# Attention on one core: keys read in place instead of through copied windows, fp32 logits in column groups, output rows gathered in SBUF and stored in 2 KB rows

## The chip, the core and the metric

The kernel runs on one core of a Trainium2 chip. The metric is the device time of one execution, in microseconds; lower is better. Engines are named as in the profile: PE (TensorE matmul), PEld (its weight loads), DVE (VectorE), ACT (ScalarE), POOL (GpSimd), SP (SyncE, which issues most DMAs here).

## What is computed

Three stages in one launch. Inputs are fp32, batch 4, 8 heads, 768 positions, head dimension 64, 8 memory keys and values a head.

```python
for c in range(768 // 32):                       # chunks of 32 queries
    k_full = concat(mem_k, k[c*32-16 : c*32+40]) # clipped at both ends
    scores = scale * q_c @ k_full.T; a = softmax(scores); out[c] = a @ v_full
x = out.transpose(0, 2, 1, 3).reshape(3072, 512)
do = x @ w_skip > 0                              # first expert stage, only these rows
e = argmax(x @ w_gate); y = gate * relu(x @ w1[e]) @ w2[e]; x = x + y
h = max(x @ v1, x @ v2, x @ v3); result = h @ w_out   # final stage, 768 wide
```

## The kernel before

**Attention.** Two heads stand on the 128 partitions, so a batch has 4 pairs (PAIRS). A pair has 768 queries: 6 tiles of 128, taken 3 at a time (TPG); such a group is one step of the pipeline, 8 steps a batch (GPB), 32 in all. Step s does, each on its engine and behind semaphores: scores of group s (PE L1034), edge mask, row maximum and subtraction (DVE L761, L764, L766), exp (ACT L629); for group s-1 the turning of the probabilities (PE L1049), their copy to probT (ACT L612), the values product (PE L1082), and on DVE the normalising (L795, L797, L801) into `xn`; for group s-2 the turning of xn (PE L1067), its split into a high part (ACT L617) and a low part (DVE L787), and the store of xn to x_dram (ACT's queue, L623); for group s-3 the logits product (PE L1060, L1061) with an 18-column weight of high and low parts. The PE order within a step is scores(s), turn prob(s-1), logits(s-3), turn xn(s-2), values(s-1). Once a batch, logits are copied (DVE L783), turned in six pieces (L1015) and summed over their two halves (DVE L749).

A score matmul has 32 queries as weights and writes 32 PSUM partitions; its moving operand is the window of both heads, 2 x 64 keys (16 left, 32 own, 8 right, 8 memory). The windows overlap, so keys are loaded to `k_raw` and copied into `k_sb`: head 0 by DVE (first half of the chunks) and POOL (second half), head 1 by ACT, in three copies each (lay_left, lay_right, L356 to L361). The other head's half of k_sb and v_sb is zero, written once: k_sb by DVE (L737 to L741), v_sb by ACT (`clear`).

**Queues.** SP loads keys one pair ahead (L382, behind the copies of the pair two back), queries (L385) and values (two DMAs, L401, behind the values product of the pair two back), with two buffers of each. The store of xn is issued by ACT in 512-byte rows, 192 KB a group, 32 in all; L800 makes DVE wait, before it writes xn, for the store of the group two back. Behind attention SP loads final weight blocks 0 and 1 (L409, EARLY), the expert chunks (L423) once the routing table stands, and the gate values.

**Routing and experts.** DVE turns the logits into a table and slot numbers (L830 to L893), POOL gathers rows of x_dram (L532), a loop over 256-row tiles follows (L1135 to L1137, split fp32 as three fp32r products), and POOL scatters the rows back (L583). ACT and DVE split weights (L654, L665, L916, L928).

**Final stage.** SP loads rows (L443, L444) and the weight blocks 2 to 5; six groups of 512 rows follow.

```python
if not isinstance(b, int) or n >= 2:          # L799, DVE
    dve.wait_ge(s_xst[g % 2], b * (16 * GPB // 2) + 16 * ((s - 1) // 2))
act.dma_start(dst[:, :, j * P:(j + 1) * P], xn[g % 2]...)   # L623
```

Of the kernel before, what the change touches and what calls it, by code (L numbers as in the profile page):

```python
# [6 lines left out]
F32 = mybir.dt.float32  # L7
F32R = mybir.dt.float32r
# [6 lines left out]
P = 128  # L15
# [3 lines left out]
WIN = LEFT + CHUNK + RIGHT + MEM  # L19
# [7 lines left out]
LOGS = LAG + 1  # L27
PADK = LEFT + S + RIGHT + MEM
GCH = NCH // GROUPS
# [14 lines left out]
W18 = 2 * (E + 1)  # L44
# [16 lines left out]
EARLY = 2  # L61


def pipeline(eng, step, ahead=False):

    for s in range(GPB):
        step(0, s)
    with eng.Fori(1, B - 1 if ahead else B) as b:  # L70
        for s in range(GPB):
            step(b, s)
    for s in range(0 if ahead else GPB, GPB + LAG):
        step(B - 1, s)


def behind(b, s, k):

    if s - k >= GPB or (isinstance(b, int) and b * GPB + s - k < 0):
        return None  # L80
    return (s - k) % GPB, b * GPB + (s - k)


def build(nc, qT, kT, vW, w9, wpack, wfin, out):
# [6 lines left out]
    with ctx:  # L91
# [12 lines left out]
        with ExitStack() as landing:  # L104

            sb, _ = tensors(landing)
            fin_raw = sb("fin_raw", [P, FB2, FC])
        sb, _ = tensors(ctx)
# [20 lines left out]
        with ExitStack() as att:  # L129
            sb, ps = tensors(att)  # L130
            q_sb = [sb(f"q_sb{i}", [P, S]) for i in range(2)]
            k_raw = [sb(f"k_raw{i}", [P, PADK]) for i in range(2)]
            k_sb = [sb(f"k_sb{i}", [P, 2, NCH, WIN]) for i in range(2)]
            v_sb = [sb(f"v_sb{i}", [P, 2, NCH, DV]) for i in range(2)]
            prob = [sb(f"prob{i}", [P, TPG, 2, WIN]) for i in range(2)]
            probT = sb("probT", [P, TPG, P])
            xn = [sb(f"xn{i}", [P, TPG, 2, D]) for i in range(2)]
            xT_hi = sb("xT_hi", [P, GW], F32R)
            xT_lo = sb("xT_lo", [P, GW], F32R)
# [3 lines left out]
            w9_sb = sb("w9_sb", [P, KD, E + 1])  # L143
            w18 = sb("w18", [P, KD, W18], F32R)
            zero = sb("zero", [P, 1])
            part = sb("part", [W18, S])
            ps_s = [ps(f"ps_s{i}", [P, TPG, 2, WIN]) for i in range(2)]

            ps_pT = ps("ps_pT", [P, GW + S // P * W18])
            ps_o = [ps(f"ps_o{i}", [P, TPG, 2, DV]) for i in range(2)]  # L150
            ps_xT = ps("ps_xT", [P, GW])
            ps_part = [ps(f"ps_part{i}", [P, GW]) for i in range(GROUPS)]
# [81 lines left out]
        s_zt = sem("s_zt")  # L234
        s_zk = sem("s_zk")
        s_zv0 = sem("s_zv0")
        s_zv1 = sem("s_zv1")
        s_w9 = sem("s_w9")
        s_q = [sem(f"s_q{i}") for i in range(2)]
        s_k = [sem(f"s_k{i}") for i in range(2)]  # L240
        s_kw = sem("s_kw")
        s_kwv = sem("s_kwv")
        s_kwa = sem("s_kwa")
        s_v = [sem(f"s_v{i}") for i in range(2)]
# [4 lines left out]
        s_carry = sem("s_carry")  # L249
# [12 lines left out]
        s_xst = [sem(f"s_xst{i}") for i in range(2)]  # L262
        s_xT = sem("s_xT")
        s_xThi = sem("s_xThi")
        s_xTlo = sem("s_xTlo")
# [4 lines left out]
        s_whi18 = sem("s_whi18")  # L270
        s_w18 = sem("s_w18")
# [58 lines left out]
        x_g = x_dram.rearrange("(b u t p) c -> b u p t c", b=B, u=GROUPS, p=P)  # L330
# [23 lines left out]
        def lay_left(copy, n, rows, head, lo, hi):  # L354
            keys = k_raw[n][:, :].rearrange("p (c w) -> p c w", w=CHUNK)
            return copy(k_sb[n][rows, head, lo:hi, 0:CHUNK], keys[rows, lo:hi, :])  # L356

        def lay_right(copy, n, rows, head, lo, hi):
            keys = k_raw[n][:, :].rearrange("p (c w) -> p c w", w=CHUNK)
            copy(k_sb[n][rows, head, lo:hi, CHUNK:WIN - MEM], keys[rows, lo + 1:hi + 1, 0:WIN - MEM - CHUNK])  # L360
            return copy(k_sb[n][rows, head, lo:hi, WIN - MEM:],  # L361
                        k_raw[n][rows, PADK - MEM:].unsqueeze(1).to_broadcast([D, hi - lo, MEM]))
# [5 lines left out]
        def _(sp):  # L368
            def one(x, b):

                return x[b] if isinstance(b, int) else x[bass.ds(b, 1)].rearrange("a p c -> (a p) c")

            def older(b, j):

                return not isinstance(b, int) or b * PAIRS + j >= 2

            def load_k(b, j):
                if older(b, j):
                    sp.wait_ge(s_kw, b * PAIRS + j - 1)
                    sp.wait_ge(s_kwa, b * PAIRS + j - 1)  # L380
                    sp.wait_ge(s_kwv, b * PAIRS + j - 1)
                sp.dma_start(k_raw[j % 2][:, :], one(kT[:, j % PAIRS], b + j // PAIRS)).then_inc(s_k[j % 2], 16)  # L382

            def load_q(b, j):
                sp.dma_start(q_sb[j % 2][:, :], one(qT[:, j], b)).then_inc(s_q[j % 2], 16)  # L385

            def load(b, s):
                j, n = s // GROUPS, s // GROUPS % 2
                if s >= GPB or s % GROUPS:
                    return  # L390

                if not (isinstance(b, int) and b == B - 1 and j == PAIRS - 1):
                    load_k(b, j + 1)
                if older(b, j):
                    sp.wait_ge(s_score, b * GPB + s - 2 * GROUPS + GROUPS)
                if not (isinstance(b, int) and b == 0 and j == 0):
                    load_q(b, j)
                if older(b, j):
                    sp.wait_ge(s_o, b * GPB + s - 2 * GROUPS + GROUPS)
                for h in range(2):  # L400
                    sp.dma_start(v_sb[n][D * h:D * h + D, h, :, :], one(vW[:, j, h], b)).then_inc(s_v[n], 16)  # L401

            load_k(0, 0)
            load_q(0, 0)
            sp.dma_start(w9_sb[:, :, :], w9).then_inc(s_w9, 16)
            pipeline(sp, load, ahead=True)
# [4 lines left out]
            sp.wait_ge(s_xn, B * GPB)  # L411
            for n in range(2):
                sp.wait_ge(s_xst[n], 16 * B * GPB // 2)
            for f in range(EARLY):
                load_fin(f)
# [61 lines left out]
        def _(pool):  # L477
# [12 lines left out]
            def windows(b, s):  # L490
                if isinstance(b, int) and b * GPB + s == 1:
                    routing_constants()
                if s >= GPB or s % GROUPS:
                    return
                j, n = s // GROUPS, s // GROUPS % 2
                pool.wait_ge(s_k[n], b * (16 * PAIRS // 2) + 16 * (j // 2 + 1))
                if not isinstance(b, int) or b * PAIRS + j >= 2:
                    pool.wait_ge(s_score, b * GPB + s - 2 * GROUPS + GROUPS)
                order()
                lay_left(pool.tensor_copy, n, slice(0, D), 0, GCH, NCH)  # L500
                lay_right(pool.tensor_copy, n, slice(0, D), 0, GCH, NCH).then_inc(s_kw, 1)
# [13 lines left out]
            pipeline(pool, windows)  # L515
            pool.wait_ge(s_logc, B)
            for n in range(2):
                pool.wait_ge(s_xst[n], 16 * B * GPB // 2)
# [8 lines left out]
            pool.wait_ge(s_route, 1)  # L527
            pool.wait_ge(s_clr, 2)
# [63 lines left out]
        def _(act):  # L592
# [3 lines left out]
            def clear(x, rows, head):  # L596
                return act_copy(x[rows, head].rearrange("p c d -> p (c d)"), zero[rows, :].to_broadcast([D, NCH * DV]))

            def windows(b, s):

                j, n = s // GROUPS, s // GROUPS % 2
                act.wait_ge(s_k[n], b * (16 * PAIRS // 2) + 16 * (j // 2 + 1))
                if not isinstance(b, int) or b * PAIRS + j >= 2:
                    act.wait_ge(s_score, b * GPB + s - GROUPS)
                lay_left(act_copy, n, slice(D, P), 1, 0, NCH)
                lay_right(act_copy, n, slice(D, P), 1, 0, NCH).then_inc(s_kwa, 1)

            def attend(b, s):
                if at := behind(b, s, 1):
                    g, n = at  # L610
                    act.wait_ge(s_pT, n + 1)
                    act.activation(probT[:, :, :].rearrange("p t c -> p (t c)"), ps_pT[:, 0:GW], ACT.Copy)\  # L612
                        .then_inc(s_pTc, 1)
# [656 lines left out]
```

## Time and profile before

| what | value |
|---|---|
| median of 3 runs | 780.99 us (779.65 to 781.51) |
| the profiled execution | 783.93 us, its span 782.2 us |
| PE busy | 725.0 us, 93% of the span |
| DVE, ACT, POOL busy | 352.6, 260.2, 115.6 us |
| mean granted clock of TensorE | 0.969 of full |
| moved | 91.35 MB; packets under 2 KB: 17644 of 40525 |

Line numbers are those of the kernel before. A fp32 matmul of the attention's scores and values products is two records in the trace (768 for 384 matmuls). Attention fills 0 to about 136 us of the span, routing up to about 160, the expert loop up to about 356, the final stage the rest. A row of a timeline gives start, duration, engine, line, what is written from what, shapes, the number of merged instructions, and in brackets the idle time before and what ended it.

### The profile page before, as it was taken

The page shows a single profiled execution, that of the slowest core. Times are in us where ns is not written, and L with a number is a line of the kernel's source. Part 1 is how long each engine was busy: PE and PEld are TensorE (multiplying, and loading weights), DVE is VectorE, ACT ScalarE, POOL GpSimd, SP SyncE. Part 2 cuts the span into 40 slices and gives each one's busy share as a digit, 9 for nine tenths or more (in the row PEclk, how much of TensorE's full clock was granted, in tenths as well). Part 3 has the DMA queues.
Part 4 walks back from the last instruction along what each step waited for, and adds up shares of the span by engine and source line. Part 5 has one row for each costly group of instructions (what it writes and reads, how often), then busy time and mean ns, then how long its engine had stood idle before and what let it go on. Part 6 is the DMA issues. An engine that isn't in the chain of part 4 may idle for free.

```text
span 782.2 us, 13009 instructions
## 1 busy us (share of the span) xinstructions
PE 725.0 (93%) x4946; PEld 596.5 (76%) x4947; DVE 352.6 (45%) x648; ACT 260.2 (33%) x414; POOL 115.6 (15%) x161
## 2 busy tenths in 40 slices
PE   4877877489999999997999999999999999999998
PEld 3665655389999999985888888888888888888886
DVE  6776887856665666662432222222222122222212
ACT  6665664245555555542321111111111111111101
POOL 3111110141545434641000000000000000000000
PEclk9999999589999999997999999999999999999999
DMA  8899895566667656637100200020030002001001
GB/s 227 222 275 264 249 287 138 193 204 198 202 211 230 205 193 208 182 110 286 44 1 1 107 1 1 11 97 1 0 108 0 0 0 107 0 0 54 1 0 54
DMA packets 40525, 91.35 MB, mean 117 GB/s; under 512 B 5356, under 2 KB 17644, under 8 KB 39728
## 3 DMA queue, kind: packets, MB, share of 16 engines
q1 hardware_dynamic: 24400, 79.67, 33.1%
q10 hardware_dynamic: 12800, 6.29, 2.8%
q0 software_dynamic: 3296, 5.00, 1.9%
q8 instruction: 19, 0.31, 0.2%
q14 instruction: 10, 0.08, 0.0%
HBM read 78.08 MB, written 16.79 MB: 121 GB/s over the span
## 4 chain that ended last, share of the span: by engine, by line
PE 81%; DMA 9%; DVE 6%; ACT 2%; issue 2%; POOL 0%; SPq 0%; ACTq 0%; DVEq 0%; POOLq 0%
PE ps_m L1135 13%; PE ps_m L1137 13%; PE ps_m L1136 13%; DMA x_dram<-xn 6%; PE ps_f L1137 4%; PE ps_f L1136 4%; PE ps_f L1135 4%; PE ps_h L1135 4%; PE ps_h L1136 4%; PE ps_h L1137 4%; PE ps_y L1135 4%; PE ps_y L1136 4%; PE ps_y L1137 4%; PE ps_fx L1179 1%; DMA q_sb<-qT 1%
## 5 line engine op out<-in xcount | busy, mean ns | idle before, releaser
L1135 PE MATMUL ps_m<-f_xhi,fin_lo 128*128 128x512 f32 x432 | 171.5, 397 | 1.4 <-DVE f_xlo L966 1.4
L1137 PE MATMUL ps_m<-f_xhi,fin_hi 128*128 128x512 f32 x432 | 171.3, 397 | 0.0
L1136 PE MATMUL ps_m<-f_xlo,fin_hi 128*128 128x512 f32 x432 | 171.3, 396 | 0.0
L916 DVE TENSOR_TENSOR w_lo<-raw,w_hi 128x1024 fp32r<-128x1024 f32 x67 | 82.9, 1238 | 62.4 <-ACT w_hi L665 62.4
L976 DVE TENSOR_TENSOR f_b<-ps_m,f_a 128x512 f32<-128x512 f32 x36 | 24.9, 692 | 181.7 <-PE ps_m L1137 181.6
L1135 PEld LDWEIGHTS ps_m<-f_xhi,fin_lo 128*128 128x128 f32 x432 | 81.6, 189 | 21.4 <-DVE f_xlo L966 1.8
L1136 PEld LDWEIGHTS ps_m<-f_xlo,fin_hi 128*128 128x128 f32 x432 | 81.6, 189 | 19.7
L1137 PEld LDWEIGHTS ps_m<-f_xhi,fin_hi 128*128 128x128 f32 x432 | 81.5, 189 | 19.8
L701 ACT ACTIVATE f_hhi<-f_h 128x512 fp32r<-128x512 f32 x36 | 22.8, 632 | 206.7 <-DVE f_h L979 206.7
L665 ACT ACTIVATE w_hi<-raw 128x1024 fp32r<-128x1024 f32 x67 | 70.9, 1058 | 56.4 <-PE ps_y L1137 50.5
L1135 PE MATMUL ps_h<-x_hi,w_lo 128*128 128x256 f32 x256 | 73.4, 287 | 2.2 <-DVE x_lo L923 2.2
L1136 PE MATMUL ps_h<-x_lo,w_hi 128*128 128x256 f32 x256 | 73.5, 287 | 0.0
L1137 PE MATMUL ps_h<-x_hi,w_hi 128*128 128x256 f32 x256 | 73.4, 287 | 0.0
L699 ACT ACTIVATE f_a<-ps_m 128x512 f32<-128x512 f32 x36 | 21.5, 596 | 113.9 <-PE ps_m L1137 113.9
L979 DVE TENSOR_TENSOR f_h<-ps_m,f_b 128x512 f32<-128x512 f32 x36 | 24.9, 692 | 75.9 <-PE ps_m L1137 75.9
L1135 PE MATMUL ps_f<-fin_hi,f_hlo 128*128 128x512 f32 x144 | 58.4, 405 | 0.0
L1137 PE MATMUL ps_f<-fin_hi,f_hhi 128*128 128x512 f32 x144 | 56.8, 394 | 0.0
L1136 PE MATMUL ps_f<-fin_lo,f_hhi 128*128 128x512 f32 x144 | 56.7, 394 | 0.0
L1135 PEld LDWEIGHTS ps_h<-x_hi,w_lo 128*128 128x128 f32 x256 | 50.0, 195 | 4.8 <-issue 2.4
L1136 PEld LDWEIGHTS ps_h<-x_lo,w_hi 128*128 128x128 f32 x256 | 50.0, 195 | 2.2
L1135 PE MATMUL ps_y<-w_hi,h_lo 128*128 128x512 f32 x128 | 51.3, 400 | 0.0
L1136 PE MATMUL ps_y<-w_lo,h_hi 128*128 128x512 f32 x128 | 50.5, 394 | 0.0
(158 smaller groups left out, 1033.6 us busy)
## 6 DMA issues: line engine op xcount, KB each, us to landing
raw<-wpack SPq DMA_DIRECT2D x67, 512.0 KB, 4.2
v_sb<-vW SPq DMA_DIRECT2D x32, 390.0 KB, 5.8
k_raw<-kT SPq DMA_DIRECT2D x16, 400.0 KB, 6.3
q_sb<-qT SPq DMA_DIRECT2D x16, 384.0 KB, 6.5
x_dram<-xn ACTq DMA_DIRECT2D x32, 192.0 KB, 4.1
fin_raw<-wfin SPq DMA_DIRECT2D x6, 1024.0 KB, 11.0
f_in<-x_dram SPq DMA_DIRECT2D x5, 1024.0 KB, 5.5
out<-f_out SPq DMA_DIRECT2D x5, 1024.0 KB, 4.2
```

The source lines that it names most:

```text
L665: act.activation(w_hi[c % RING][:, :], raw[:, c % RAW, :], ACT.Copy).then_inc(s_whi, 1)
L699: act.activation(f_a[:, :], ps_m[0][:, :], ACT.Copy).then_inc(s_fa, 1)
L701: act.activation(f_hhi[f % 2][:, :], f_h[:, :], ACT.Copy).then_inc(s_fhhi, 1)
L916: dve.tensor_tensor(w_lo[c % RING][:, :], raw[:, c % RAW, :], w_hi[c % RING][:, :].bitcast(F32), ALU.subtract).then_inc(s_wlo, 1)
L976: dve.tensor_tensor(f_b[:, :], ps_m[1][:, :], f_a[:, :], ALU.max).then_inc(s_fb, 1)
L979: dve.tensor_tensor(f_h[:, :], ps_m[2][:, :], f_b[:, :], ALU.max).then_inc(s_fh, 1)
L1135: pe.matmul(out_, a_lo, b_hi, start=first, stop=False)
L1136: pe.matmul(out_, a_hi, b_lo, start=False, stop=False)
L1137: return pe.matmul(out_, a_hi, b_hi, start=False, stop=end)
L1179: last = pe.transpose(ps_fx[:, t * P:(t + 1) * P], f_in[par][:, t, k * P:(k + 1) * P], ident[:, :])
```

## The change

- Keys: no k_raw and no copies. k_sb holds the 800 raw columns of both heads (the other head's rows zero). A score is two matmuls, one over 2 x 56 keys read in place, one over 2 x 8 memory keys. Keys land by two DMAs of 64 partitions.
- Three buffers of q, k, v (SETS) instead of two. SP issues all loads in order, keys and queries of the next pair behind the values of this one.
- Output: DVE writes the normalised rows into `x_buf`, which holds all of x (24 tiles of 512 columns). SP stores it once a batch, 1.5 MB, batches 0 to 2 after all loads of attention, then final weight block 0, then batch 3. No store on ACT's queue, and no wait of DVE for one.
- Logits: xT is copied once by ACT in fp32, with no low part. Three matmuls (one a tile) with a 32-column weight, each to its own 32 PSUM partitions. They are copied, turned in one piece and copied to `logits` once a group of the last pair, 8 times.
- POOL clears v_sb and then writes the routing constants; ACT does no clearing. The loops over batches are unrolled.
- Waits on the stores move: POOL before the gather, ACT before its first final split (x_buf and fin_hi share their place). Final block 1 is loaded behind the first rows of the final stage.

```diff
-            q_sb = [sb(f"q_sb{i}", [P, S]) for i in range(2)]
-            k_raw = [sb(f"k_raw{i}", [P, PADK]) for i in range(2)]
-            k_sb = [sb(f"k_sb{i}", [P, 2, NCH, WIN]) for i in range(2)]
+            q_sb = [sb(f"q_sb{i}", [P, S]) for i in range(SETS)]
+            k_sb = [sb(f"k_sb{i}", [P, 2, PADK]) for i in range(SETS)]
...
+            def load_qk(n):
+                b, j, i = n // PAIRS, n % PAIRS, n % SETS
+                if n >= SETS:
+                    sp.wait_ge(s_score, (n - SETS + 1) * GROUPS)
+                for h in range(2):
+                    sp.dma_start(k_sb[i][D * h:D * h + D, h, :], kT[b, j, D * h:D * h + D, :]).then_inc(s_qk[i], 16)
+                sp.dma_start(q_sb[i][:, :], qT[b, j]).then_inc(s_qk[i], 16)
+
+            def load_v(n):
+                b, j, i = n // PAIRS, n % PAIRS, n % SETS
+                if n >= SETS:
+                    sp.wait_ge(s_o, (n - SETS + 1) * GROUPS)
+                for h in range(2):
+                    sp.dma_start(v_sb[i][D * h:D * h + D, h, :, :], vW[b, j, h]).then_inc(s_v[i], 16)
+
+            def store_x(b):
+                sp.wait_ge(s_xn, (b + 1) * GPB)
+                sp.dma_start(x_b[b], x_buf[:, b * (S // P):(b + 1) * (S // P), :]).then_inc(s_xst, 16)
...
+            load_qk(0)
+            sp.dma_start(w9_sb[:, :, :], w9).then_inc(s_w9, 16)
+            for n in range(NPAIR):
+                load_v(n)
+                if n + 1 < NPAIR:
+                    load_qk(n + 1)
+            for b in range(B - 1):
+                store_x(b)
+            load_fin(0)
+            store_x(B - 1)
...
+            load_fin(1)
             sp.dma_start(f_in[1][:, :, :], x_f[1]).then_inc(s_fin[1], 16)
-            for f in range(EARLY, FB2):
+            for f in range(2, FB2):
...
+            pool.wait_ge(s_xst, 16 * B)
             pool.wait_ge(s_clr, 2)
...
-                    act.activation(xT_hi[:, :], ps_xT[:, :], ACT.Copy).then_inc(s_xThi, 1)
+                    act_copy(xT[:, :], ps_xT[:, :]).then_inc(s_xTc, 1)
...
+            act.wait_ge(s_xst, 16 * B)
             split_fin(0)
...
-                    dve.wait_ge(s_xThi, n + 1)
-                    dve.tensor_tensor(xT_lo[:, :], ps_xT[:, :], xT_hi[:, :].bitcast(F32), ALU.subtract)\
-                        .then_inc(s_xTlo, 1)
...
-                    if not isinstance(b, int) or n >= 2:
-                        dve.wait_ge(s_xst[g % 2], b * (16 * GPB // 2) + 16 * ((s - 1) // 2))
...
-                            last = pe.matmul(ps_s[g % 2][CHUNK * r:CHUNK * (r + 1), t, :, :],
-                                             q_sb[j % 2][:, c * CHUNK:(c + 1) * CHUNK],
-                                             k_sb[j % 2][:, :, c, :], start=True, stop=True)
+                            queries = q_sb[i][:, c * CHUNK:(c + 1) * CHUNK]
+                            rows = slice(CHUNK * r, CHUNK * (r + 1))
+                            pe.matmul(ps_s[n % 2][rows, t, :, 0:KEYS], queries,
+                                      k_sb[i][:, :, c * CHUNK:c * CHUNK + KEYS], start=True, stop=True)
+                            last = pe.matmul(ps_s[n % 2][rows, t, :, KEYS:], queries,
+                                             k_sb[i][:, :, PADK - MEM:], start=True, stop=True)
...
-                    pe.matmul(ps_part[u][0:W18, :], w18[:, j, :], xT_lo[:, :], start=(j == 0), stop=False)
-                    pe.matmul(ps_part[u][0:W18, :], w18[:, j, :], xT_hi[:, :], start=False,
-                              stop=(j == PAIRS - 1)).then_inc(s_part, 1)
+                    for t in range(TPG):
+                        last = pe.matmul(ps_part[u][t * W9:(t + 1) * W9, 0:P], w9_sb[:, j, :], xT[:, t * P:(t + 1) * P],
+                                         start=(j == 0), stop=(j == PAIRS - 1))
+                    last.then_inc(s_part, 1)
```

## Rows read from the trace of the kernel before

**Rows 1.** The page's part 4: chain that ended last, by engine
```profile
PE 81%; DMA 9%; DVE 6%; ACT 2%; issue 2%; POOL 0%; SPq 0%; ACTq 0%; DVEq 0%; POOLq 0%
```

**Rows 2.** The chain in 20 to 136 us: by line; start, us, what
```profile
by line: DMA x_dram<-xn 41.4%; issue 7.1%; ACT k_sb L594 7.1%; DVE xn L801 5.1%; PE ps_xT L1067 4.5%; DVE smax L764 4.4%; PE ps_s L1034 4.4%; DVE prob L766 3.9%; PE ps_o L1082 3.7%; DVE xT_lo L787 3.4%; PE ps_pT L1049 3.0%; ACT xT_hi L617 1
...
70.09 7.91 DMA x_dram<-xn
```

**Rows 3.** Groups by line, DVE, 0 to 136 us: busy, mean ns, idle
```profile
L801 DVE TENSOR_TENSOR xn<-ps_o,srec 128x384 f32<-128x384 f32 x32 | 17.8, 558 | 15.7 <-DMA x_dram<-xn 14.4
...
L787 DVE TENSOR_TENSOR xT_lo<-ps_xT,xT_hi 128x384 fp32r<-128x384 f32 x32 | 17.5, 546 | 3.4 <-ACT xT_hi L617 3.2
```

**Rows 4.** Queues in 0:20, 20:60, 60:120, 120:134: packets, MB, engine share
```profile
q1 hardware_dynamic: 1468, 4.43, 83.6%
...
q1 hardware_dynamic: 2242, 8.02, 73.8%
q10 hardware_dynamic: 4175, 2.06, 18.0%
...
q1 hardware_dynamic: 3442, 12.40, 75.9%
q10 hardware_dynamic: 6625, 3.25, 18.5%
...
q1 hardware_dynamic: 160, 0.80, 25.8%
```

**Rows 5.** Busy by window: five engines, PE clock, DMA share, GB/s
```profile
50.00:60.00 10.00, 8.58 (x174) 6.50 (x174) 8.63 (x28) 6.86 (x13) 1.20 (x4) 1.00 1.01 282
```

**Rows 6.** Timeline of PE, 33 and 116 to 127 us: start, us, what
```profile
33.01 1.52 PE L1034 MATMUL ps_s<-k_sb,q_sb 128*32 128x128 f32 x24
...
116.50 0.55 PE L1015 MATMUL ps_pT<-ident,part 18*128 18x18 f32 x6
...
122.20 0.86 PE L1034 MATMUL ps_s<-k_sb,q_sb 128*32 128x128 f32 x24
...
124.84 0.84 PE L1034 MATMUL ps_s<-k_sb,q_sb 128*32 128x128 f32 x24
125.61 0.55 PE L1049 MATMUL ps_pT<-ident,prob 128*128 128x128 f32 x3
125.91 0.42 PE L1060 MATMUL ps_part<-xT_lo,w 128*18 128x384 f32 x1
...
126.83 0.87 PE L1082 MATMUL ps_o<-v_sb,probT 128*32 128x130 f32 x24
```

**Rows 7.** Groups by line, PE, 115 to 127 us: busy, mean ns
```profile
L1034 PE MATMUL ps_s<-k_sb,q_sb 128*32 128x128 f32 x96 | 3.4, 272 | 0.0
...
L1015 PE MATMUL ps_pT<-ident,part 18*128 18x18 f32 x6 | 0.5, 214 | 0.0
```

**Rows 8.** Timeline of the start: weights of the first values product
```profile
13.13 1.09 PEld L1082 LDWEIGHTS ps_o<-v_sb,probT 128*32 128x32 f32 x24 [1.70 <-DMA v_sb<-vW]
```

**Rows 9.** Timeline from the logits to the first expert product
```profile
135.38 0.27 DVE L749 TENSOR_REDUCE logits<-ps_pT 128x54 f32<-128x108 f32 x1 [0.98 <-PE ps_pT L1015]
...
135.71 0.95 POOL L520 MEMSET x_in<- 128x1024 f32 x1 [22.44 <-DVE logits L749]
...
151.72 1.21 POOL L532 DMA_INDIRECT x_in<-x_dram,idx_g  x1 [0.29 <-POOL idx_g L537]
...
159.84 0.57 PE L1135 MATMUL ps_h<-x_hi,w_lo 128*128 128x256 f32 x1 [2.19 <-DVE x_lo L923]
```

**Rows 10.** The page's part 6, DMA issues: count, KB each, us to landing
```profile
fin_raw<-wfin SPq DMA_DIRECT2D x6, 1024.0 KB, 11.0
...
out<-f_out SPq DMA_DIRECT2D x5, 1024.0 KB, 4.2
```

**Rows 11.** Timeline of ACT at the start of the final stage
```profile
364.68 1.90 ACT L654 ACTIVATE fin_hi<-fin_raw 128x2048 fp32r<-128x2048 f32 x1
370.57 0.60 ACT L699 ACTIVATE f_a<-ps_m 128x512 f32<-128x512 f32 x1 [3.99 <-PE ps_m L1137]
```

More of the change, by code:

```diff
@@ L26 @@
 LAG = 3
-LOGS = LAG + 1
+STEPS = B * GPB
+NPAIR = B * PAIRS
+SETS = 3
 PADK = LEFT + S + RIGHT + MEM
-GCH = NCH // GROUPS
 GW = TPG * P
@@ L60, with pipeline @@
 NIX = 2
[L61 to L81, printed above, removed]
+def pipeline(step):
+    for s in range(STEPS + LAG):
+        step(s)
 def build(nc, qT, kT, vW, w9, wpack, wfin, out):
@@ L261, in build @@
         s_xn = sem("s_xn")
-        s_xst = [sem(f"s_xst{i}") for i in range(2)]
+        s_xst = sem("s_xst")
         s_xT = sem("s_xT")
-        s_xThi = sem("s_xThi")
-        s_xTlo = sem("s_xTlo")
+        s_xTc = sem("s_xTc")
         s_part = sem("s_part")
@@ L352, in first_rows, with where, spot @@
             return x[:, :, t * P:(t + 1) * P]
[L354 to L362, printed above, removed]
+        def where(n):
+            return n // GPB, n % GPB // GROUPS, n % GROUPS
+        def spot(n):
+            return n // GPB * (S // P) + n % GROUPS * TPG
         block = ctx.enter_context(nc.Block())
@@ L513, in routing_constants @@
                               allow_small_or_imprecise_dtypes=True).then_inc(s_rc, 1)
[L515 to L518, printed above, removed]
+            pool.wait_ge(s_const, 1)
+            for i in range(SETS):
+                for h in range(2):
+                    if 2 * i + h > 0:
+                        pool.wait_ge(s_zv, 2 * i + h)
+                    pool.memset(v_sb[i][D * h:D * h + D, 1 - h, :, :], 0.0).then_inc(s_zv, 1)
+            pool.wait_ge(s_zv, 2 * SETS)
+            routing_constants()
+            pool.wait_ge(s_logc, B * GROUPS)
             pool.memset(x_in[:, :, :], 0.0).then_inc(s_clr, 1)
@@ L644, in _ @@
-            act.wait_ge(s_w9, 16)
-            act.activation(w18[:, :, 0:E + 1], w9_sb[:, :, :], ACT.Copy).then_inc(s_whi18, 1)
-            clear(v_sb[1], slice(0, D), 1)
-            pipeline(act, attend, ahead=True)
+            pipeline(attend)
             act.wait_ge(s_ldiff, 1)
@@ L752, in attend @@
-            def attend(b, s):
-                if at := behind(b, s, 0):
-                    g, n = at
+            for i in range(SETS):
+                for h in range(2):
+                    dve.memset(k_sb[i][D * h:D * h + D, 1 - h, :], 0.0).then_inc(s_zk, 1)
+            def copy_logits(n):
+                dve.wait_ge(s_log, n + 1)
+                dve.tensor_copy(logits[:, n * TPG:(n + 1) * TPG, :],
+                                ps_part[n % GROUPS][:, P:].rearrange("p (t e) -> p t e", e=W9)[:, :, 0:E + 1])\
+                    .then_inc(s_logc, 1)
@@ L789, in attend @@
-                if s == LOGS and not (isinstance(b, int) and b == 0):
-                    copy_logits(b)
-                if at := behind(b, s, 1):
-                    g, n = at
+                if 0 <= (n := s - 3) < STEPS:
+                    b, j, u = where(n)
+                    if j == PAIRS - 1:
+                        dve.wait_ge(s_part, n + 1)
+                        dve.tensor_copy(part[:, u, :], ps_part[u][0:TPG * W9, 0:P]).then_inc(s_partc, 1)
+                if 0 <= (n := s - 1) < STEPS:
+                    b, j, u = where(n)
```

299 lines of the change are left out of this document (89 added, 210 removed).

## The prediction

> **What bounds the kernel now.** I read the chain of work that ended last first. Over the whole span it is 81% matmul and 9% DMA [rows 1]; the matmuls belong to the two expert stages after about 160 us, and the change leaves their code alone. So the gain or loss must come from the attention stage, 0 to 136 us, and from what it hands on. The same chain, cut to 20 to 136 us, is another picture: 41.4% of it is the store of normalised rows, `x_dram<-xn`, in pieces of up to 7.91 us [rows 2]. With two `xn` buffers, the multiply of group n (L801) waits until the store of group n-2 has landed: DVE stands 14.4 us before it [rows 3].
>
> Why does a 192 KB store take 6 to 8 us? The queues answer. In 20 to 60 us the loads (q1) take 73.8% of the 16 engines and the stores (q10) 18.0%; in 60 to 120 us 75.9% and 18.5% [rows 4]. In 50 to 60 us their busy share is 1.01, at 282 GB/s [rows 5]. **The DMA engines are nearly full, and a small store queues among big loads.** The chain names the store's latency; the resource behind it is engine time. That decides the estimate: removing the wait can bring the stage down to the engine time of its loads, and no further.
>
> **What the loads need.** Their engine time is 83.6% of 20 us, 73.8% of 40, 75.9% of 60 and 25.8% of 14 [rows 4]: 16.7 + 29.5 + 45.5 + 3.6 = 95.3 us. Bytes of q, k and v are the same afterwards. The stores take 18.0% of 40 and 18.5% of 60, 18.3 us up to 120, and some 3 more behind; three quarters of them now go behind the last load, the rest behind those. Loads start at about 2 us and can hold the engines full, since the first three pairs (SETS = 3) wait for nothing and later ones only for a pair three back. So the last values land at about 2 + 95.3 = 97 us, and the last keys and queries, ahead of that half pair of bytes, at about 94 to 95.
>
> **What the compute needs.** In the one stretch without store waits, score bursts start at 122.20 and 124.84: 2.64 us a group [rows 6]. Inside it two hand-offs lock the step: from 125.61 to 126.83 PE turns prob, ACT copies it to probT, and the values product may start (1.22); the values burst follows, and the next score burst. The parts:
> - Scores: 12 matmuls over 128 columns become 24, over 112 and 16. Each fp32 matmul is two records: 24 records become 48. The four 32-column groups run side by side now: a record of 128 columns takes 0.27 us, and 24 take 0.84 [rows 6, 7]. Total columns stay, so the low end of the cost is zero. The nearest row for a small fp32 matmul is the turn of `part` (L1015, 18 columns, six in 0.55 us, one 0.21): (0.55 - 0.21) / 5, about 68 ns each [rows 6, 7]. Over four column groups at once, six added records each, that is 0.41 us, less the 0.07 that the shorter key matmuls give back: 0.34. L1015 loads 128 weight columns, these 32, so I take 0.25. The high end is all 24 added records one after another, 1.63 us.
> - Logits: one pair of 384-column matmuls (L1060 and L1061; the record of the first alone is 0.42 us [rows 6]) becomes three matmuls in three column groups, six records of 128 columns; two rounds of about 0.11 us, 0.25 with the hand-over. PE gains 0.2 us, but that stretch lies beside ACT's probT copy, which sets the start of the values product: nothing on the path.
> - DVE loses xT_lo, 0.546 us a group [rows 3], and its key copies; it gets logits copies 8 times instead of 4, small ones. ACT loses its key copies and the 32 store issues. Neither engine then has 2.6 us of work in a group. POOL's copies go too. All of that is hidden under PE and DMA and counts zero; it only makes the 2.64 safe.
> - SP loses all waits for copied windows (three semaphores) and gains the four stores of x, placed behind all loads. What queues behind a store's wait on SP is the first final weight block, then the first expert chunks, due later.
> So a group costs 2.64 + 0.25 = 2.89 us of compute, against 95.3 / 32 = 2.98 us of DMA. **DMA is the bound by a little**, and compute follows the loads.
>
> **The start.** The first values product came at 13.13, waiting for v, which stood behind the next pair's keys in the queue [rows 8]. Now the scores wait for k, q and two memsets, no window copies (about 5 us, an estimate), and v(0) comes directly behind: about 9.5. POOL clears v_sb instead of ACT: by x_in's 0.95 us for 1024 columns [rows 9], 1.45 us each, two before the first product, all six by 11 us: hidden by the loads. Pair 1 lands at about 12.
>
> **The sum.** Last pair's scores at 95, the last group's at 98. From the last score burst (124.84) to the end of the logits reduction (135.38 + 0.27) is 10.8 us now [rows 6, 9]; without xT_lo, with a copy of 128 instead of 384 columns and one turn of logits instead of six, about 9.5. That gives 107.5; I add 2 us for loads that don't pack perfectly: logits at **109.5** instead of 135.65, 26.1 us earlier. Routing (135.65 to the gather at 151.72, 16.1 us) and the way on to the first expert product (159.84) are the same code [rows 9]. Everything behind shifts, if the stores don't hold it.
>
> **The stores of x.** SP reaches them near 87 us; they flow from 97. Three of 1.5 MB, 1 MB of final weights, and the last 1.5 MB: some 7.3 MB. At 282 GB/s [rows 5] they need 26 us and end at 123. The gather is due at 109.5 + 16.1 = 125.6: 2.6 us of slack. At the 4.2 us to landing that a 1 MB store has [rows 10], one by one, it would be 128, 2 us late; that is an upper bound, since these overlap. I count zero and keep 2 to 5 us for the range. ACT now waits for these stores before it splits the first final block; then come 1.9 us and three splits of half the elements each, about 1 us, to about 128, before the first expert product (109.5 + 24.2 = 133.7).
>
> **The final stage.** Final block 1 now lands behind f_in[0], and such a block takes 11.0 us from issue to landing among others [rows 10], that is about 368.5 on the old clock. Its split (1.90 us, at 364.68 now) stands in front of f_a at 370.57, which has 4.0 us of idle before it [rows 11]: it just fits. Zero, and 1 us for the range.
>
> The profiled execution took 783.93 us; 783.93 - 26.1 = 757.8. It lies 2.9 above the median of the runs, so I predict 780.99 - 26.1 = **754.9, rounded 755**. Its own range, with 0 to 0.34 us a group for the small matmuls and loads 6% better or worse, is 750 to 761.
>
> **Rivals.**
> (1) *The score burst is paced by its records, not its columns.* 24 records in 0.84 us, less the 0.27 of one, are 25 ns each [rows 6, 7]; that fits a fixed pace too. Then 48 records add 0.6 us, a group costs 3.24, and from pair 1 at 12 us the last score burst is at 12 + 29 x 3.24 = 106, logits at 115 to 117: gain 19 to 21, 761. For it: those rows alone don't separate the two readings. Against it: a burst at the lower clock took 1.52 us [rows 6], nearly twice as long, as column work must and a fixed pace of issue needn't. Chance 0.2.
> The Trainium skill has this rule (TensorEngine Tiling (Array Packing), Instruction Overhead): every matmul carries about 60 cycles, so one column costs as much as sixty, and splitting a dimension that is already small doesn't pay. By it the 24 small records cost an estimated 25 ns each, 0.6 us a group if they line up, and the result is this rival's 761; spread over four column groups it would be 0.15, within my term.
> (2) *Slower: the small matmuls serialise.* If each record of the memory matmuls holds up its column group's neighbours for L1015's 68 ns, the score burst grows by 1.6 us, a group takes 4.27, the last score burst comes at 12 + 29 x 4.27 = 136 and the logits at 145: about 10 us later than now, 791. The turn is at 3.94 us a group, 54 ns for each added record. For it: L1015 is the only small fp32 matmul in the trace. Against it: it loads four times the weight columns, in no column group. Chance 0.06.
> (3) *The DMA bound stays or moves.* Keys now land by two DMAs of 64 partitions, as v does; if the loads run 8% slower, or the stores come 5 us late for the gather, the gain is 18 to 21: 760 to 763. Chance 0.12.
> (4) *Nothing comes of it*: the stage is bound by something that I don't see, and stays within 2 us. Chance 0.03.
> The forecast has the remaining 0.59.
>
> **How the numbers follow.** The range 749 to 768 holds the forecast, rivals 1 and 3 with some room, and leaves out 2 and 4. Faster by over 0.3% (2.3 us, about what this kernel's measurement can tell from no change): 0.91; within it 0.03; slower 0.06.
>
> **What would show it.** DMA share near 1.0 from 3 to 97 us with no stores in it; no L801 wait on a DMA; PE waiting for q, k or v at pair starts; a score burst of 0.9 to 1.2 us (1.4 means rival 1, over 2 rival 2); groups at 2.9 to 3.0 us; logits ready at 107 to 112; the gather with no wait for stores; the expert stages as long as before. PE without idle through the stage, at over 3.1 us a group, would say that compute and not DMA is the bound, and my term for the small matmuls is wrong. A span of expert stages that differs by over 2 us would be a cause that I haven't counted.

## The result and the profile after

The change made the kernel slower: 797.9 us (median of 4 runs, 793.3 to 800.3) against 781.3 for the kernel before on the same chip, a ratio of 1.019 [1.012, 1.027]. 755 was predicted, and the range ended at 768. The page of the changed kernel's profiled execution (793.31 us, the shortest of the four, 4.6 below their median), its span, PE's busy time and the DMA queues:

```profile
span 791.5 us, 14338 instructions
...
PE 731.7 (92%) x5827; PEld 605.0 (76%) x5827; DVE 325.1 (41%) x572; ACT 224.8 (28%) x361; POOL 109.3 (14%) x119
...
q1 hardware_dynamic: 27792, 86.01, 36.2%
...
q8 instruction: 33, 0.54, 0.3%
...
q_sb<-qT SPq DMA_DIRECT2D x16, 384.0 KB, 7.6
```

q8 is of the kind "instruction". The page of the kernel before has for it:

```profile
q8 instruction: 19, 0.31, 0.2%
```

The change writes PE's 32 attention groups out one after another where the kernel before loops over batches, and PE's compiled program grew from 313 KB to 546 KB. q8's packets are of 16 KB, and in both kernels their sum is the size of PE's program: they are its blocks, fetched.

The timeline between attention and the experts (lmax, DVE's first step on the finished logits; the gather; the first expert product) answers to [rows 9]:

```profile
146.24 0.35 DVE L716 TENSOR_REDUCE lmax<-logits 128x24 f32<-128x192 f32 x1
...
162.27 1.21 POOL L483 DMA_INDIRECT x_in<-x_dram,idx_g  x1 [0.29 <-POOL idx_g L488]
...
170.43 0.58 PE L1013 MATMUL ps_h<-x_hi,w_lo 128*128 128x256 f32 x1 [2.20 <-DVE x_lo L807]
```

The same DVE step (L830 there) began at 135.69 before. So the logits are done 10.6 us **later**, not 26 earlier. From there on nothing differs much: 16.0 us to the gather and 8.2 to the first product, as before, and the 9.3 us by which the span is longer are these 10.6 less 1.3 behind. In this execution the whole loss is in attention; where the other 4.6 us of the median lie, no trace shows.

Now PE's timeline there. One group is as forecast; the next is cut in two:

```profile
65.09 0.41 PE L909 MATMUL ps_s<-k_sb,q_sb 128*32 128x112 f32 x8
...
66.02 0.55 PE L921 MATMUL ps_pT<-ident,prob 128*128 128x128 f32 x3
...
67.32 0.87 PE L956 MATMUL ps_o<-v_sb,probT 128*32 128x130 f32 x24
68.02 0.40 PE L909 MATMUL ps_s<-k_sb,q_sb 128*32 128x112 f32 x6
68.20 0.24 PE L911 MATMUL ps_s<-k_sb,q_sb 128*32 128x16 f32 x4
70.01 0.18 PE L911 MATMUL ps_s<-k_sb,q_sb 128*32 128x16 f32 x1 [1.56 <-issue]
```

The reader is to see two things. From burst to burst it is 68.02 - 65.09 = 2.93 us, against my 2.89; the burst to the turn of prob takes 0.93, against 0.77 before (124.84 to 125.61 [rows 6]): 24 added records cost 0.16 us. Then PE stops in the middle of a burst for 1.56 us, with its operands in place. "issue" is idle time for which the profile shows no releaser. PE's rows of this kind in the waits of 0 to 150 us:

```profile
PE ps_s L909 <- issue: 9.1, 5, 2.9
PE ps_s L911 <- issue: 6.0, 3, 3.1
PE ps_o L956 <- issue: 5.0, 1, 5.0
PE ps_part L932 <- issue: 4.1, 3, 1.4
PE ps_pT L921 <- issue: 2.1, 1, 2.1
```

They sum to 26.3 us. In the trace's packets the 16 KB fetches of q8 come every 4 to 9 us from 27 to 141 us and take 0.9 to 1.5 us each. Of PE's 13 stops of over 1 us behind 18 us, nine begin 0.9 to 1.5 us after such a packet starts, that is about when it ends, and three more have a whole packet inside them. So the stops stand at the fetches, but what PE waits for inside one, the rest of this block or the next, the trace doesn't show. In the kernel before there were 7 fetches up to 73 us and none from there to 160. DVE's two longest waits are on PE now, none on a DMA: the store wait of [rows 3] is gone, and something took its place.

### The profile page after: what moved, and what is told of

It is laid out like the page before. It is cut to its first block, busy times and chain, and to the rows that moved or that the text cites. A ratio compares the mean times of both kernels' runs of the same rounds, so it can differ in the third digit from the quotient of the medians.

```text
span 791.5 us, 14338 instructions
## 1 busy us (share of the span) xinstructions
PE 731.7 (92%) x5827; PEld 605.0 (76%) x5827; DVE 325.1 (41%) x572; ACT 224.8 (28%) x361; POOL 109.3 (14%) x119
## 4 chain that ended last, share of the span: by engine, by line
PE 65%; DMA 2%; issue 0%; POOL 0%; DVE 0%; SPq 0%; ACT 0%; POOLq 0%; DVEq 0%
PE ps_m L1013 13%; PE ps_m L1014 13%; PE ps_m L1015 13%; PE ps_f L1015 4%; PE ps_f L1014 4%; PE ps_f L1013 4%; PE ps_y L1013 2%; PE ps_y L1014 2%; PE ps_h L1015 2%; PE ps_h L1014 2%; PE ps_y L1015 2%; PE ps_h L1013 2%; PE ps_fx L1057 1%; DMA x_in<-x_dram,idx_g 1%; DMA f_in<-x_dram 1%; PE ps_x L1007 1%
```

## The experiments

**Theory F (fetch):** written out, PE uses up 16 KB of program in fewer microseconds than a block needs to be there while q1 fills the DMA engines, and it runs dry. **Rivals:** the 24 small score records (W); the split key loads that make transfers slower (D); the three-deep load queue that makes the fetches wait (Q); and that the store part saves nothing. The kilobytes of PE's program are those of the compiled kernel; the packets of q8 bear them out (26 in e1, 22 in e5, 33 in e6). Times are medians; ratios are to the kernel before in the same batch.

### e1: the kernel before, PE's attention written out

```diff
-            pipeline(pe, attend)
+            for n in range(B):
+                for s in range(GPB):
+                    attend(n, s)
+            for s in range(GPB, GPB + LAG):
+                attend(B - 1, s)
```

> The kernel before, with PE's attention written out for all four batches instead of looping over three of them; every instruction, operand and wait is the same. PE's program grows from 313 KB to 429 KB, some 7 fetches of 16 KB more while the DMA engines are full. Theory F (PE stalls while its instructions are fetched through full DMA engines): slower by 5 to 15 us, 786 to 796, partly hidden behind the store waits. Rival W (the small matmuls and the added PE work make the change slow): no difference, 781. Rival D (the loads of the changed kernel are slower): no difference, 781.

784.0 us, 1.005 [1.001, 1.009]. A small cost, under what F had expected: either the store waits hide the gaps, or a 429 KB program is fetched in time. e11 tells these apart. PE has no row with "issue" in its attention, so even the 0.5% isn't explained by stops.

### e2: the change without its later loads

```diff
             (load_qk and load_v, from the fourth pair on)
+                    return
-                        pe.wait_ge(s_qk[i], 48 * (p // SETS + 1))
+                        pe.wait_ge(s_qk[i], 48)
```

> The changed kernel, that loads q, k and v for the first three pairs alone and uses them for all 16 (13 of 16 loads are left out); PE's program is the same to the byte. F: fetches pass an idle queue, the idle of PE put down to issue falls from about 26 us to under 8, groups take 2.9 us, 750 to 762. W: the same PE work at the same pace, 790 to 798. D predicts a gain too, but with the issue stalls still there: 785.

790.0 us, but the total can't be compared: other values route the rows differently, and 75 expert blocks are loaded instead of 67. Attention can: lmax at 117.83, 28.4 us earlier. Its queues and PE's issue rows in 20 to 110 us:

```profile
q1 hardware_dynamic: 2592, 6.19, 20.0%
q8 instruction: 19, 0.31, 1.4%
...
PE ps_s L911 <- issue: 2.6, 1, 2.6
PE ps_s L913 <- issue: 1.3, 1, 1.3
PE ps_pT L923 <- issue: 1.2, 1, 1.2
```

The same program is fetched, 19 blocks in 90 us, one in 4.7 us, and PE stops for 5.1 us; in the change it was 15 blocks and 17.5 us in the same stretch. The three stops of e2 end at 20.4 us and begin at 71.1 and 99.2: the first beside the first three pairs' loads (DMA share 1.05 in 15.0 to 20.4 us), the other two 1 and 3 us after the last packet of a stored batch of x (0.54 in 64 to 72 us, 0.53 in 96.0 to 100.5). So the fetches alone don't stall PE for long; **it takes the fetches and nearly full DMA engines together**. Part of the 28 us is also that PE no longer waits for loads, which this run doesn't separate.

### e3, e4: fewer instructions a group

e3 drops the memory keys' matmuls (12 of 128 columns a group, PE's program 447 KB). e4 computes the same as the change, but with one full-width matmul of 16 columns for each tile, 3 a group in place of 12 (472 KB):

```diff
-                            last = pe.matmul(ps_s[n % 2][rows, t, :, KEYS:], queries,
-                                             k_sb[i][:, :, PADK - MEM:], start=True, stop=True)
+                    for t in range(TPG):
+                        last = pe.matmul(ps_s[n % 2][:, t, :, KEYS:], q_sb[i][:, c:c + P],
+                                         k_sb[i][:, :, PADK - MEM:], start=True, stop=True)
```

> The changed kernel with one score matmul over 2 x 64 columns read in place (the 8 columns behind the window in place of the 8 memory keys, which are left out). 48 instructions a group less on PE, program 447 KB instead of 546 KB, 6 fetches fewer. F: 13 to 18 us faster than the change, 780 to 785, with issue stalls left. W: the whole loss and the missed gain come back, 755 to 760. D: unchanged, 797.

> The changed kernel with the memory keys of a whole tile of 128 queries in one matmul (3 of full width a group instead of 12 of 32 columns), same result. 36 instructions a group less, program 472 KB, 4.6 fetches fewer. F: 7 to 12 us faster than the change, 786 to 791. W: most of the loss back, 760 to 770. D: unchanged, 797.

e3: 773.9 us (five runs; the profiled one took 784.3, the others 768.4 to 775.4), 0.989 [0.984, 0.994], 24 us below the change where 13 to 18 were expected. 24 fewer records save some 32 x 0.16 = 5 us by their own time, an estimate; that the rest is stalls isn't shown, since the one trace is of the longest execution. It has 17.3 us of "issue" in 0 to 150 us against the change's 26.3, with a program of 7.8 KB a group, and in 20 to 110 us the DMA share of 0.99 that I had forecast for the change:

```profile
20.00:110.00 90.00, 73.43 (x1419) 50.44 (x1419) 51.36 (x153) 33.41 (x71) 0.00 (x0) 0.96 0.99 227
```

e4: 788.1 us, 1.006 [1.003, 1.010], 9.8 below the change and inside what F expected (7 to 12), though an undisturbed group takes 0.4 us longer with it. A group that is slower by itself, but has fewer bytes (8.6 KB in place of 10.9), made the kernel faster. PE's "issue" rows fell to 6.4 us, all before 73 us.

### e5, e6, e10, e7: loop or written out, the changed kernel

e5 loops PE over the batches again. With it come two load sets instead of three (a batch has four pairs), and two xn buffers into which DVE writes and which ScalarE copies into x_buf. e6 is e5 with the loop written out, and nothing else. e10 is e5 with that copy on GpSimd. e7 is the change with two sets alone.

```diff
-            pipeline(attend)
+            for s in range(GPB):
+                attend(0, s)
+            with pe.Fori(1, B) as b:
+                for s in range(GPB):
+                    attend(b, s)
```

> The changed kernel with two sets of q, k, v instead of three and PE's attention looping over batches 1 to 3, as before the change. [...] Program 371 KB instead of 546 KB. F: issue stalls after the first loop round are gone, groups of 2.9 to 3.1 us behind it, 15 to 25 us faster than e6 (the same written out). If a loop body of 86 KB doesn't stay with PE, fetches go on and there is no difference. W: no difference to e6.

> As e5, with PE's attention written out: program 546 KB, 23 fetches. F: 795 to 802. W: the same time as e5.

> The changed kernel with two sets of q, k, v instead of three, nothing else. F: the third set was worth little where PE is late, 797 to 803. Rival Q (deeper load queues make the instruction fetches wait longer): fewer issue stalls, 785 to 793. D: 800 to 806, since loads wait more.

> The change with PE's attention as a loop over batches and two sets (the run of 779.2 us), with the copy of the rows moved from ScalarE to GpSimd, which is idle in attention. Theory (that run is bound in attention by its loads and by PE's first batches, not by ScalarE): total within 2 us of 779, logits at 127 to 130. Rival (ScalarE's copy behind the last store, 7.8 us of waiting there, holds the chain up): 3 to 6 us less, 773 to 776.

e5: 779.2 us, 0.997 [0.994, 1.000]. e6: 793.3, 1.015 [1.008, 1.022]. **The same work costs 14.1 us more when PE's code is written out**, as F has it, though F had expected 15 to 25. The instruction queue and the window of 73 to 117 us, first e5, whose loop is running there, then e6:

```profile
73.00:117.00 44.00, 41.09 (x1143) 31.58 (x1146) 29.74 (x90) 24.84 (x55) 0.00 (x0) 1.00 0.99 238
```

```profile
q8 instruction: 7, 0.11, 1.2%
...
PE ps_s L925 <- issue: 2.9, 1, 2.9
PE ps_s L927 <- issue: 2.7, 1, 2.7
PE ps_part L949 <- issue: 1.9, 1, 1.9
PE ps_pT L938 <- issue: 1.0, 1, 1.0
...
73.00:117.00 44.00, 35.54 (x833) 26.58 (x837) 22.13 (x67) 18.08 (x40) 0.00 (x0) 0.88 0.82 197
```

In e5 there is no q8 packet in this window and no PE row with "issue"; PE is busy for 41.1 of 44 us and the DMA share is 0.99. In e6 both fall, PE to 35.5 and the DMA share to 0.82: PE is late, buffers come free late, and the loads then idle.

A stop costs more than its idle time. In e6 the granted clock of TensorE falls to half, 1.2 GHz, at 75.6, 96.0 and 113.1 us, each time less than 1 us behind a stop; the first of these stretches:

```profile
75.60:79.00 3.40, 3.40 (x56) 2.55 (x59) 0.36 (x3) 1.31 (x3) 0.00 (x0) 0.50 0.18 56
```

Over the window it is 0.88, and 1.00 in e5. PE's 833 records take 35.54 us there, 43 ns each, against 36 ns in e5; so some 5 to 6 us of the window go to the slower clock, an estimate, beside 8.5 us of stops.

e5 isn't free of stops either. Its batch 0 is written out and the first round of its loop has to be fetched too; the last such fetch starts at 71.5 us, the next at 129.6. Up to 73 us it has 9.9 us of "issue" (e6 8.3), behind it none (e6 10.4). The largest rows of 0 to 73 us:

```profile
PE ps_s L927 <- issue: 2.5, 2, 1.5
PE ps_s L925 <- issue: 2.4, 1, 2.4
PE ps_pT L938 <- issue: 2.0, 1, 2.0
```

So the 14.1 us are the price of writing out 16 more groups, not all that the fetches cost.

e7: 790.5, 1.011 [1.007, 1.014], outside what F expected (797 to 803) and inside Q's 785 to 793. But its stops are as long as the change's (18.3 us in 20 to 110 us, 17.5 there), the intervals of the two overlap, and e6 with the same two sets is at 793: the third set didn't help, and whether it harmed is open. e10: 779.4, 0.999 [0.997, 1.002]: ScalarE's copy was not in the way.

### e8, e12: the keys by one transfer over 128 partitions

```diff
-                for h in range(2):
-                    sp.dma_start(k_sb[i][D * h:D * h + D, h, :], kT[b, j, D * h:D * h + D, :]).then_inc(s_qk[i], 16)
+                sp.dma_start(k_sb[i][:, 0, :], kT[b, j]).then_inc(s_qk[i], 16)
```

> The changed kernel with keys loaded by one DMA of 128 partitions instead of two of 64 (head 1's keys land in head 0's columns, so the head's separation is left out; bytes, matmuls and program are the same). D: q packets go back from 185 to 132 ns and the loads' engine time from 105 to 95 us, and the stage is 8 to 10 us shorter. F: the engine time may fall, the time by at most 4 us, because PE is late and not the loads.

> The change with two sets and PE's loop (779.2 us, logits at 129.0), and the keys loaded by one transfer over 128 partitions in place of two over 64 (the separation of the heads in the keys is left out of the computation, so the scores of both heads mix). With PE written out the same edit gave 2.7 us, not told from noise. Theory (with PE looped, the loads' engine time, 105 us against 95, is what binds the groups behind the first batch): 5 to 9 us less, total 770 to 774, logits at 120 to 124. Rival (the copies, the column-group burst and the steady 2.9 us of compute bind it): 0 to 3 us less, 776 to 779.

e8 (in the change): 795.2, 1.018 [1.009, 1.026], not told from the change. e12 (in e5): 775.9, 0.991 [0.988, 0.995], 3.3 us below e5 by the medians and 0.6% by the ratios, whose intervals just touch (e5: 0.994 to 1.000); lmax at 124.89 against 129.00. That is less than the 5 to 9 us expected, and nearer to the rival's 0 to 3. Queue q1 in 20 to 110 us, e5 and then e12:

```profile
q1 hardware_dynamic: 5611, 19.43, 89.2%
```

```profile
q1 hardware_dynamic: 5548, 19.72, 83.6%
```

89.2% of 90 us for 19.43 MB is 4.13 us a MB, 83.6% for 19.72 is 3.82. By the packets it is the queries that pay most: a 3072 B packet of q takes 185 ns in the change and 127 in e8, 132 before; one of 3200 B of the keys takes 210, 194 and 186. The loads became slower, and that costs 3 to 5 us once PE keeps up; while PE stalls, it costs nothing that e8 could show.

### e9, e11: the store part alone, looped and written out

e9 is the kernel before with one part of the change: GpSimd copies each xn into x_buf, and SP stores 2 KB rows once a batch; the loads of the final blocks and the waits on the stores move as in the change.

```diff
-                    act.dma_start(dst[:, :, j * P:(j + 1) * P], xn[g % 2][:, :, :, :].rearrange("p t h d -> p t (h d)"))\
-                        .then_inc(s_xst[g % 2], 16)
+                    pool.tensor_copy(dst, xn[g % 2][:, :, :, :].rearrange("p t h d -> p t (h d)")).then_inc(s_xc, 1)
...
+                sp.dma_start(x_b[b], x_buf[:, b * (S // P):(b + 1) * (S // P), :]).then_inc(s_xst, 16)
```

> The kernel before with the store part of the change alone: PE's attention stays the loop over batches, the key windows, the copied keys and the fp32r logits stay, but GpSimd copies each normalised group from its two buffers into rows kept in SBUF and SyncE stores them once a batch in 2 KB rows, in place of ScalarE's 32 stores of 512 B rows that the next normalisations waited for. Theory (the store part is worth what the prediction said, and the change lost it to PE's instruction fetches and to longer loads): the waits of DVE on a DMA go, logits end at 112 to 120 us in place of 135, and the total is 760 to 768 us. Rival (the store waits only covered the same engine time of loads and PE work, as the groups of the looped run with two sets, 2.9 to 3.4 us each, suggest): logits at 124 to 130, total 772 to 777. Second rival (GpSimd's copies of 128x256 fp32, which compete with DVE's reads, become the new wait): no gain, 779 to 785, with DVE waiting on POOL.

> The kernel before with the store part (the run of 770.3 us, whose logits are done at 121.3 us) and PE's attention written out step by step in place of the loop; nothing else differs. Written out alone, with the store waits of before still there, it cost 2.4 us. Theory (fetches of a written-out program stall PE, and the store waits hid most of that in the kernel before): without those waits it costs 5 to 12 us, total 775 to 782, logits at 126 to 133, fetches on the instruction queue through all of attention. Rival (only the 24 added records a group make the program long enough to matter): 1 to 3 us, total 771 to 774.

e9: 770.3 us, 0.989 [0.984, 0.994]. lmax is at 121.32, 14.4 us earlier. DVE's normalisation, which answers to the first line of [rows 3]:

```profile
L814 DVE TENSOR_TENSOR xn<-ps_o,srec 128x384 f32<-128x384 f32 x32 | 17.8, 558 | 1.3
```

Its idle fell from 15.7 us to 1.3. **The store part is real and worth some 10 us** (5 to 13 by the interval), where 13 to 21 were expected; it beats both kernels. e11: 770.0, 0.985 [0.981, 0.988]: written out, at 7.3 KB of code a group, it costs nothing that these runs can tell, and PE has no row with "issue". So my expectation for e11 (5 to 12 us) was wrong, and e1's explanation is the second: this program is fetched in time, one block in some 7 us.

### e13 to e16: the same kernel with more bytes

If bytes decide, e11 must become slow when it is given the change's bytes. e13 and e14 add 112 waits a group that are satisfied already, to e9 and e11.

> The kernel before with the store part and PE's loop (770.3 us), with 112 more instructions a group on PE, each a wait for a semaphore that was reached long ago, put ahead of the wait for prob; PE's program becomes 370 KB, the size of the changed kernel's loop with two sets. This is the control: it shows what the filling costs by being worked through. Both theories: 770 to 776 us, since PE waits there for the softmax in part anyway; what it is above 770 is the price of working through the filling.

> The same filling in the written-out program (770.0 us without it); PE's program becomes 544 KB, as in the change, with 10.9 KB of instructions a group. Theory (fetches of a program that is used faster than about 16 KB in 4 to 5 us stall PE while the DMA engines are full): 8 to 16 us above the filled loop, idle of PE put down to issue in mid-group, fetches every 4 to 5 us. Rival (the 14 us of the changed kernel hang on something else in it): within 3 us of the filled loop.

e13: 965.1 us, 1.232 [1.228, 1.235]. e14: 964.0, 1.229 [1.225, 1.233]. Both were expected under 795, and they decide nothing: the filling cost 195 us, the groups became three times as long, so a block came only every 14 us, beside a q1 share of 33%. PE in e13, before one turn of prob:

```profile
157.31 0.90 PE L1064 MATMUL ps_pT<-ident,prob 128*128 128x128 f32 x3 [4.67 <-issue]
```

These 4.67 us over 112 waits are 42 ns for one. 195 us over 32 x 112 are 54 ns, which is an upper bound, since the granted clock also fell (0.67 in 20 to 110 us, 0.98 in e9). e15 and e16 add bytes that take little time: each score matmul of e9 and e11 is cut in two, as in the change.

```diff
+                            for w in (slice(0, 56), slice(56, 64)):
-                                             k_sb[j % 2][:, :, c, :], start=True, stop=True)
+                                                 k_sb[j % 2][:, :, c, w], start=True, stop=True)
```

> The kernel before with the store part and PE's loop (770.3 us), each score matmul cut into one of 112 and one of 16 columns, with the same result; PE's program is 362 KB. It is the price of the added records without the fetches. Theory: 0.16 us a group for 24 added records, as in the change, so 3 to 7 us at most: 770 to 777. Rival (the records cost more than that, and are the loss of the change): 780 or more.

> The same cut in the written-out program (770.0 us without it); PE's program is 527 KB, 10.3 KB of instructions a group. Theory (PE is stalled by fetches when it uses 16 KB in less than about 5 us beside full DMA engines): 6 to 14 us above the looped one, with PE idle put down to issue inside the score bursts. Rival (the 14 us of the changed kernel hang on something else in it): within 3 us of the looped one.

e15 (looped): 774.5, 0.991 [0.988, 0.995], 4 us over e9. e16 (written out): 780.7, 0.999 [0.996, 1.002], 6.2 us over e15, at the low end of the 6 to 14 expected; lmax at 133.84 against 124.20 (both traces are from the far ends of their runs, 783.6 and 771.0 us). The issue rows of 20 to 125 us and q8 in 73 to 117, of e16:

```profile
PE ps_s L1047 <- issue: 4.3, 2, 3.2
PE ps_o L1095 <- issue: 1.6, 1, 1.6
PE ps_xT L1080 <- issue: 1.0, 1, 1.0
...
q8 instruction: 7, 0.11, 1.1%
```

In e15 no q8 packet falls into that window. But the rows don't divide e16's loss cleanly. e15 has 5.3 us of "issue" too, all before 73 us while its first 16 groups are fetched; behind that e16 has one stop of 3.2 us and e15 none. PE's wait for q grew from 1.7 to 7.0 us, and what makes q late there is not shown. The difference of the medians is the price of writing out, since nothing else differs; how it comes about is read better from e5 and e6.

**Written out costs 0 us at 7.3 KB a group (e11), 6 at 10.3 KB with groups of 3.3 us (e16), 14 at 10.9 KB with groups of 2.9 (e6).** That is shown in two kernels with different keys, copies and logits, so it is the code and not another part of the change.

## Why the prediction was wrong

- **The step that failed** is "a group costs 2.64 + 0.25 = 2.89 us of compute, against 95.3 / 32 = 2.98 us of DMA. DMA is the bound by a little". Both terms describe work; PE's own instructions stand in neither. The diff showed the loop over batches gone, and the page showed q8; I costed that edit at nothing and didn't name it. It is worth 14 us (e5 against e6), of the 24 (by the ratios) to 28 us between the store part alone (770) and the change (798), and stops of the first 16 groups, 9.9 us in e5, come on top.
- **The loads**: "bytes of q, k and v are the same afterwards" is right, but the engine time isn't. q1 took 45.5 us for 12.40 MB, 3.67 us a MB [rows 4]; in the change it is 4.16 (85.8% of 20 to 110 us for 18.56 MB, no store among them), in e5 4.13. That makes the term of 95.3 us, 2.98 a group, about 106 and 3.3, an estimate. Rival 3 named this cause, but as a loss of up to 8% from a gain; it is 12 to 13% a MB. The split keys cost 3 to 5 us (e12). By itself it moves the sum from 755 to about 766, an estimate and still in the range.
- **The small matmuls** were right: 0.16 us a group in the timeline where I took 0.25. e15's total, 4 us over e9 (0.2% by the ratios), holds their time and its 5.3 us of stops together. Rivals 1 and 2 both fall: the burst to the turn took 0.93 us, not 1.4 and not over 2. 0.16 us over 24 records are 7 ns each, or 27 ns for each of the six that one column group gets. The Trainium skill's rule (TensorEngine Tiling (Array Packing), Instruction Overhead) of about 60 cycles a matmul, an estimated 25 ns, would give 0.6 us if the records lined up and 0.15 spread over four column groups; the trace agrees with the second.
- **The store part** was right in kind: the L801 wait on a DMA went, no later one took its place, and the gather waited for no store. Its size was over-read. I let the stage fall to the loads' engine time; alone it gives 10 us in the total and 14 at lmax (e9). Behind the waits PE, DVE and the DMA engines are all nearly full (39.2 and 39.4 of 44 us and a share of 0.94 in 73 to 117 us); which of them binds, no run tells.
- **The start** was a little off: the first scores came at 6.08, not about 5, the first values product at 11.36, not 9.5, and pair 1's scores at 13.43, not 12, with 0.5 us of waiting for q.
- **"Slower" had 0.06**, and by another mechanism. The turn that I had put at 3.94 us a group was passed (by the trace's starts of DVE's maximum over the scores, 31 steps take 4.2 us each, 3.8 before), but by stops of 1.2 to 5 us and not by small matmuls that hold each other up. The row that would have warned me was q8's.

The sum of the parts, in ratios to the kernel before: store part -1.1%; keys in place with a looped PE +0.9% (e9 to e5), of it 0.6% the split key loads, and with e5's 9.9 us of stops inside it, where e9 has none; PE written out +1.7% (e5 to e6); the change against e6 +0.5%, inside both intervals. The remaining 0.3% is about what the split scores cost alone, 0.2% (e9 to e15). The runs are from several chips, each beside its own runs of the kernel before, so these small differences are good to some tenths of a per cent. It wasn't tried at what share of busy DMA engines the stalls begin; there are two points only, q1 at 20% and at 76% and more.

## What to carry to other kernels

Price an engine's program like a load: bytes of code a step (here 7 to 11 KB for a group of 3 us) against the time of that step, and look at the page's instruction queue before a hot loop is written out beside DMA engines that are nearly full. Where they are too many, keep the loop, or cut instructions, even where each remaining one takes longer (e4); at 7.3 KB a group of 3.3 us writing out cost nothing here (e11). And test a many-part change part by part: one part of this one gave 10 us, and the others took them and 17 more.

## What the runs showed of the hardware

- PE's instruction fetch shares the DMA engines: 16 KB packets that take 0.9 to 1.5 us, and beside a q1 share of 76% and more stops of 1 to 5 us each. A program of 7.3 KB a group of 3.3 us, a block in 7.4 us, had none (e11); from 8.6 KB a group of 3.3 us, a block in 6.3 us (e4: 6.4 us of stops), up to 10.9 KB in 2.9 us, a block in 4.4 us (the change: 26.3 us) they were there. These are three points of different kernels and no rule. A loop of eight groups fetched its code in its first round; in the second and third e5 and e15 fetched nothing and e9 one block.
- The Trainium skill (Runtime: NRT & Kernel Launch, Instruction fetch mechanics) says that 16 KiB blocks are fetched ahead, that crossing one is "mostly hidden" and that kernels prefer full unrolling where possible. The block size agrees. "Mostly hidden" holds here with nearly idle DMA engines (e2) or sparse code (e11) and not in the change; full unrolling brought nothing here (e1, e11) or cost 6 to 14 us (e16, e6).
- The granted clock fell to half behind stops of 1.9 to 2.9 us (e6, at 75.6, 96.0 and 113.1 us), so such a stop costs more than it lasts.
- A semaphore wait that is already satisfied took PE 42 ns by one gap and at most 54 by e13's total.
- The 3072 B packets of q, a load over 128 partitions, took 185 ns when the keys beside them came by two loads of 64 partitions, and 127 to 132 when by one of 128 (e8, before). The values came by two loads of 64 partitions in both.
